# Attention with a two-part fp32r product with V, nine blocks per two heads, six narrow MLP tiles mixed in, written out without loops

## The reference

```python
scores = scale * np.matmul(q, k.transpose(0, 1, 3, 2))
thresh = np.max(scores, axis=-1, keepdims=True) - tau
scores = np.where(scores >= thresh, scores, -1000000000.0)
scores = scores - np.max(scores, axis=-1, keepdims=True)
attn = np.exp(scores)
attn = attn / (np.sum(attn, axis=-1, keepdims=True) + 1e-09)
out = np.matmul(attn, v)
# x: [2304, 512]
h = x @ w_in;  g = h * np.clip(h + 3.0, 0.0, 6.0) / 6.0;  x = g @ w_out
h = x @ w2_in; g = h * (1.0 / (1.0 + np.exp(-1.702 * h))); out = g @ w2_out
```

## Time and profile before

| | before |
|---|---|
| median of 3 runs | 1230.28 us |
| profiled execution, its span | 1225.6 us |
| PE busy (modelled ends) | 1184.3 us, 97% |
| PEld busy | 1020.1 us, 83% |
| DVE busy | 525.8 us, 43% |
| ACT busy | 563.2 us, 46% |
| POOL busy | 545.1 us, 44% |
| chain that ended last | PE 86%, DVE 4%, ACT 4%, issue 4% |
| PE's first product | 11.5 us |
| the first tile behind the attention | from 524.8 us |

### The profile page before, as it was taken

One profiled execution on the slowest core, in us unless ns is written; L12 is line 12 of the kernel. 1 busy time (PEld: TensorE's weight loads), 2 busy tenths in 40 slices (PEclk: granted clock), 3 DMA queues, 4 the chain that ended last, 5 costly groups with the idle time before them and its releaser, 6 DMA issues.

```text
span 1225.6 us, 19677 instructions
## 1 busy us (share of the span) xinstructions
PE 1184.3 (97%) x6408; PEld 1020.1 (83%) x6408; DVE 525.8 (43%) x1344; ACT 563.2 (46%) x1002; POOL 545.1 (44%) x457
## 2 busy tenths in 40 slices
PE   5999999989998999989999999999999999999998
PEld 3666677757776677789999999999999999999997
DVE  5777765576656766332222222222222322222221
ACT  5888765566645765444323333233333222222221
POOL 5888655456645565345333333224444222222222
PEclk9999999999999999999999999999999999999999
DMA  4333322141222312323233322112222112222210
GB/s 121 93 103 111 85 58 60 30 118 49 58 58 68 94 35 58 88 68 120 86 113 111 111 102 81 42 57 72 86 86 86 52 52 78 78 77 77 77 52 26
DMA packets 69736, 94.29 MB, mean 77 GB/s; under 512 B 24368, under 2 KB 45872, under 8 KB 69680
## 3 DMA queue, kind: packets, MB, share of 16 engines
q1 hardware_dynamic: 69680, 93.62, 24.8%
HBM read 70.01 MB, written 23.59 MB: 76 GB/s over the span
## 4 chain that ended last, share of the span: by engine, by line
PE 86%; DVE 4%; ACT 4%; issue 4%; POOL 0%; DMA 0%; DVEq 0%; ACTq 0%; SPq 0%; POOLq 0%
PE mm L417 19%; PE score L429 16%; PE tr L417 14%; PE score L427 12%; PE mm L403 10%; PE score L381 5%; PE tr L389 5%; PE mm L427 5%; ACT expd L663 2%; DVE neg_max L537 2%; DVE prob L551 1%; ACT w_hi L684 1%; ACT gate L702 1%; DVE act_f L580 1%; ACT x_hi L698 0%
## 5 line engine op out<-in xcount | busy, mean ns | idle before, releaser
L814 POOL TENSOR_TENSOR g_lo<-act_f,g_hi 128x384 fp32r<-128x384 f32 x192 | 193.8, 1014 | 442.8 <-ACT g_hi L710 442.8
L803 POOL TENSOR_TENSOR prob<-prob,inv_total 128x576 f32<-128x576 f32 x160 | 183.3, 1148 | 179.5 <-DVE inv_total L565 179.1
L403 PE MATMUL mm<-pt,v_raw 128*64 128x320 f32 (+1 forms) x640 | 182.4, 416 | 4.3 <-ACT o_t L678 4.3
L669 ACT ACTIVATE pt<-tr 128x640 f32<-128x640 f32 x160 | 112.3, 702 | 101.1 <-PE tr L389 100.1
L417 PE MATMUL mm<-x_hi,w_hi 128*128 128x384 f32 x432 | 149.6, 346 | 5.7 <-DVE x_lo L572 3.1
L551 DVE SCALAR_TENSOR_TENSOR prob<-score,thresh,expd 128x576 f32<-128x576 f32 x160 | 130.2, 813 | 50.4 <-ACT expd L663 43.7
L663 ACT ACTIVATE expd<-score,neg_max 128x576 f32<-128x576 f32 x161 | 118.9, 739 | 57.4 <-DVE neg_max L537 56.2
L417 PE MATMUL mm<-x_hi,w_lo 128*128 128x384 f32 x432 | 144.8, 335 | 0.0
L417 PE MATMUL mm<-x_lo,w_hi 128*128 128x384 f32 x432 | 144.7, 335 | 0.0
L537 DVE TENSOR_REDUCE neg_max<-score 128x1 f32<-128x576 f32 x161 | 121.5, 755 | 38.8 <-PE score L381 38.5
L403 PEld LDWEIGHTS mm<-pt,v_raw 128*64 128x64 f32 x640 | 77.1, 136 | 68.1 <-issue 22.0
(11 more groups left out here) (64 smaller groups left out, 2266.8 us busy)
## 6 DMA issues: line engine op xcount, KB each, us to landing
x_raw<-x_t_scratch SPq DMA_DIRECT2D x24, 768.0 KB, 5.8
q_raw<-in_qT SPq DMA_DIRECT2D x68, 144.0 KB, 2.8
k_raw<-in_kT SPq DMA_DIRECT2D x68, 144.0 KB, 2.9
stage<-in_w_in SPq DMA_DIRECT2D x16, 512.0 KB, 6.4
stage<-in_w_out SPq DMA_DIRECT2D x16, 512.0 KB, 6.5
x_t_scratch<-o_t SPq DMA_DIRECT2D x32, 144.0 KB, 2.4
part_t_scratch<-y_out SPq DMA_DIRECT2D x6, 768.0 KB, 4.2
part<-part_t_scratch SPq DMA_DIRECT2D x6, 768.0 KB, 7.8
```

Of the source, the lines that this page charges most:

```text
L403: m = pe.matmul(pv_out[0:HD, 0:n_q], v_raw[:, par, c, :], pt[:, c, cols], start=c == 0, stop=c == QB - 1)
L669: act.activation(pt[:, :, j * P:j * P + P], turned_p.rearrange("p (c n) -> p c n", c=QB), ACT.Copy).then_inc(pt_copied, 1)
L803: pool.tensor_tensor(p, p, inv_total[:, s % RING:s % RING + 1].broadcast_to([P, S]), ALU.mult).then_inc(norm_done, 1)
L814: pool.tensor_tensor(g_lo[:, c, :], act_f[:, c % 2, :], g_hi[:, c, :], ALU.subtract).then_inc(g_lo_done, 1)
```

## The change

A pair of heads now takes nine slots: blocks 0 to 3 of the first head, one block (MID = 4) that holds the last 64 queries of both heads (eight score products, four of them for each head, since q_sp holds zeros beside each tail), and four blocks of the second head. 144 slots in all (G). What each engine does in slot g:

```diff
-            def prob_v(head, par, group, chunks):
...
-                    m = pe.matmul(pv_out[0:HD, 0:n_q], v_raw[:, par, c, :], pt[:, c, cols],
+            def prob_v(n, low):
+                k, side = n % 4, (n % 4) // 2
+                width = GROUP_COLS[k][1]
+                if not low:
+                    pe.wait_ge(pt_hi_done, group_last(n) + 1)
+                    pe.wait_ge(v_lo_done, 2 * (n // 4) + side + 1)
+                    wait(pe, merged, n)
+                else:
+                    wait_low(pe, group_last(n))
+                for c in range(CHUNKS):
+                    p_part = (pt_hi, pt_lo)[low]
+                    m = pe.matmul(pv_out[:, 0:width], v_hl[:, side, c, :], p_part[:, GROUP_BUF[k], c, 0:width],
+                                  start=not low and c == 0, stop=low and c == CHUNKS - 1)
```

v_hl holds V's high part in 64 columns and its low part in the other 64, so one bank receives both parts for 128 rows. The groups are 256, 320, 320 and 256 queries wide. ScalarE copies the lower half out and VectorE adds it to the upper half (`merge`). The tables say in which slot of a pair (counted on past 8) each group's three steps stand:

```diff
+    PV_HI = {4: 0, 7: 1, 9: 2, 11: 3}
+    PV_LO = {5: 0, 8: 1, 10: 2, 12: 3}
+    MERGE = {6: 0, 9: 1, 11: 2, 13: 3}
+    BY_POOL = (5, 8)
```

PE's program:

```diff
+            for g in range(END):
+                if g + 2 < G:
+                    scores(g + 2)
+                if 0 <= g - 2 < G:
+                    turn(g - 2)
+                n = at_slot(PV_HI, g)
+                if n is not None:
+                    prob_v(n, False)
+                n = at_slot(PV_LO, g)
+                if n is not None:
+                    prob_v(n, True)
+                if g in PIECE:
+                    mixed_piece(*PIECE[g])
```

VectorE's program:

```diff
+            for g in range(END):
+                done = PIECE.get(g - 1)
...
+                        gated(ti, mix_out, p).then_inc(mix_drained, 1)
...
+                        drain_y(ti, mix_out, (p - FC) // 2).then_inc(mix_drained, 1)
+                if g + 2 < G:
+                    row_max(g + 2)
+                if g + 1 < G:
+                    mask(g + 1)
+                    if (g + 1) % 2:
+                        invert((g + 1) // 2)
+                if 0 <= g - 2 < G and kind(g - 2) not in BY_POOL:
+                    low_turned(g - 2)
+                n = at_slot(MERGE, g)
+                if n is not None:
+                    merge(n)
```

MLP mixing: step 0 is cut into eight tiles of 288 tokens, and six of them run inside, in pieces of 12 products (a chunk of h, or half a y block):

```diff
+    for b in range(1, B):
+        g0, every = BATCH_SLOTS * b + SLOTS + 1, 8 if b + 1 < B else 4
+        for p in range(2 * PIECES):
+            PIECE[g0 + p + p // every] = (2 * (b - 1) + p // PIECES, p % PIECES)
```

More of the change, by code:

```diff
@@ new lines, in pool_blocks, with wait_low, pt_place @@
+        def pool_blocks(x):
+            return sum(kind(y) in BY_POOL for y in range(x))
+        POOLED = [pool_blocks(x) for x in range(G + 1)]
+        def wait_low(eng, x):
+            wait(eng, lo_by_dve, x + 1 - POOLED[x + 1])
+            wait(eng, lo_by_pool, POOLED[x + 1])
+        def pt_place(tile, x):
+            s = kind(x)
+            if s != MID:
+                group, col = PLACE[s]
+                return tile[:, GROUP_BUF[group], :, col:col + P]
+            base = tile[:, 0, :, 2 * P:2 * P + TAIL]
+            after = tile[:, 1, :, 0:TAIL]
+            return bass.AP(tensor=base.tensor, offset=base.offset,
+                           ap=[list(base.ap[0]), list(base.ap[1]), [after.offset - base.offset, 2], list(base.ap[2])])
@@ L584, in drain_y, with low_turned, merge @@
-            def drain_y(step, bank, m, tile):
+            def low_turned(x):
+                dve.wait_ge(pt_hi_done, x + 1)
+                dve.tensor_tensor(pt_place(pt_lo, x), turned_place(x), pt_place(pt_hi, x), ALU.subtract
+                                  ).then_inc(lo_by_dve, 1)
+            def merge(n):
+                width = GROUP_COLS[n % 4][1]
+                dve.wait_ge(o_low_done, n + 1)
+                wait(dve, o_stored[n % 2], 16 * (n // 2))
+                dve.tensor_tensor(o_t[:, n % 2, 0:width], pv_out[0:HD, 0:width], o_low[:, 0:width], ALU.add
+                                  ).then_inc(merged, 1)
@@ L591, in drain_y @@
                 if partial is None:
-                    return dve.tensor_scalar(y_part(y_out, step, m), bank, scale, None, ALU.mult)
-                return dve.scalar_tensor_tensor(out=y_part(y_out, step, m), in0=bank, scalar=scale,
-                                                in1=y_part(part, step, m), op0=ALU.mult, op1=ALU.add)
-            def pair(i, unit, mlp):
-                for s in range(SLOTS):
-                    g = SLOTS * i + s
-                    mask(g, s)
-                    row_max(g + 1, s + 1)
-                    threshold(g + 1, s + 1)
-                    sum_total(g, s)
-                    if mlp is not None:
-                        mlp(s)
-                    invert(g, s)
@@ L621, in _ @@
-            attention(dve, pair, mix)
-            for k in range(KC):
-                low_x(MIXED, k)
-            def tile_body(step, tile, units):
-                base = first_item(step, tile)
+                    return dve.tensor_scalar(y_part(y_out, ti, m), bank, scale, None, ALU.mult)
+                return dve.scalar_tensor_tensor(out=y_part(y_out, ti, m), in0=bank, scalar=scale,
+                                                in1=y_part(part, ti, m), op0=ALU.mult, op1=ALU.add)
+            row_max(0)
@@ L696, in high_x, with high_half_unit @@
+            def high_half_unit(step, u, n):
+                act.wait_ge((win_loaded, wout_loaded)[n], 16 * (UNITS * step + u + 1))
+                col = n * UNITS * UNIT + u * UNIT
+                act.activation(w_hi[step % 2][:, col:col + UNIT], stage[:, n, :], ACT.Copy).then_inc(w_hi_done, 1)
+            def high_x(ti, k):
+                width = TILES[ti][2]
                 if k == 0:
[L697 to L698 removed]
@@ L700, in gates @@
-            def gates(step, bank, c):
+                    act.wait_ge(x_loaded, 16 * (ti + 1))
+                act.activation(x_hi[:, k, 0:width], x_raw[:, k, 0:width], ACT.Copy).then_inc(x_hi_done, 1)
+            def gates(ti, bank, c):
+                step, _, width = TILES[ti]
                 if step < 2:
-                    act.activation(gate[:, c % 2, :], bank[:, 0:TT], ACT.Relu, bias=three[:, :]
+                    act.activation(gate[:, c % 2, 0:width], bank[:, 0:width], ACT.Relu, bias=three[:, :]
@@ L782, in _ @@
+                high_g(ti, FC - 1)
+                if ti + 1 < len(TILES):
+                    for k in range(KC):
+                        high_x(ti + 1, k)
+                for n in range(2):
+                    if ti == MIXED:
+                        high_half_unit(1, 2, n)
+                    if step > 0 and t < UNITS and step + 1 < STEPS:
+                        high_half_unit(step + 1, t, n)
         @block.gpsimd
@@ L835, in mix @@
-            def mix(tile, s):
-                if s in SPLIT_G:
-                    low_g(SPLIT_G[s], tile)
-            attention(pool, pair, mix)
-            def tile_body(step, tile, units):
-                for c in range(FC):
-                    low_g(c, tile)
-                for unit in units:
-                    for n in range(2):
-                        low_unit(step + 1, unit, (step + 1) * UNITS + unit, n)
-            for step in range(STEPS):
-                tiles_of(pool, step, tile_body)
+            low_q(0)
```

984 lines of the change are left out of this document (513 added, 471 removed).

## The result

| | before | after |
|---|---|---|
| median of 4 runs each | 1230.45 us (1229.63 to 1230.89) | 1394.12 us (1390.92 to 1395.94) |
| ratio | | 1.133, 95% interval 1.131 to 1.135 |
| span of the profiled execution | 1225.6 us | 1389.0 us |
| Pool busy | 545.1 us, 44% | 731.4 us, 53% |

A forecast was written before the change was run, and what follows sets the result against it. TensorE was taken as the bound, except VectorE's chain in attention slots without MLP work. Terms 14.5, 149, 434, 30, 60.6 and 600.7 gave 1289 us of span; with 4.7 for the median, 1293 us, 5% slower, range 1240 to 1335.

The forecast's parts named there:

- bare slots: Slots 0 to 45 of the attention, without MLP work: 13 with the wait at 4.7, 33 at 2.65, 149 us.
- mixed slots: Slots 46 to 143 of the attention, with MLP pieces mixed in: four kinds of slot, together 434 us.
- to the first narrow tile: Slots 144 to 157: 11 MLP pieces, the last turns and PV, three drains of one bank: 30 us.
- two narrow tiles: Two MLP tiles behind the attention: 51.1 us, and 9.5 of stalls while step 1's weights are staged, 60.6 together.
- steps 1 to 3: MLP steps from the fourth tile's start to the end, untouched by the change: 600.7 us.
- The wait: TensorE's high products with V wait for VectorE's merge of the group before, on one bank: 2.7 us in 45 places.
- the clock: Rival: waits drop TensorE to 1.2 GHz in bare slots, PE work doubles: 50 us more, 1343 us; chance 0.08.
- the trace of before speaks against it: Argument against the lower clock: the granted clock is 1.00 in every stage of the kernel before.
- the terms 6.6, 4.7 and 3.7: Length in us of mixed slots: 6.6 with wait and MLP piece, 4.7 with wait alone, 3.7 with piece alone.
- Edits at nothing: Pool's threshold and normalize, unrolling, single q, k, v buffers cost nothing; Pool 28 us a pair against 30, hidden.
- The term of 2.65 us: Slot without MLP work or merge wait, paced by VectorE's sum: about 2.65 us, bounds 2.3 and 3.1.
- The first rival: The merge falls early enough or other slots catch up, so its wait costs nothing: 1179 us, 4% faster; chance 0.15.

The follow-up runs named there:

- fill: Changed kernel plus 20 unread TensorE products of 224 columns ahead of high products that wait for the merge, where the bank is free: 1356.6 us, ratio 1.104.
- merge_first: Changed kernel with VectorE's merge and ScalarE's copy of the lower half at the head of their slots: 1261.0 us, ratio 1.026.
- k_w_moved: merge_first plus one-element sums, broadcast-tensor normalize, step 1 weights staged elsewhere, and k_lo and attention weight splits in other slots: 1221.2 us, ratio 0.992.
- norm_tt: Changed kernel with Pool's normalize as a product with a broadcast tensor instead of tensor_scalar: 1379.3 us, ratio 1.124.
- merge_mid: k_w_moved with VectorE's merge behind the row maximum of block g+2 instead of at the slot's head: 1244.4 us, ratio 1.011.
- merge_norm: merge_first with Pool's normalize as a product with a broadcast tensor: 1263.4 us, ratio 1.028.

## Why the prediction was right in direction and wrong in size

By its own sum, the span (predicted 1289, measured 1389.0):

| stretch | predicted | measured |
|---|---|---|
| to the first mask | 14.5 | 13.7 |
| bare slots | 149 | 188.6 |
| mixed slots | 434 | 490.0 |
| to the first narrow tile | 30 | 32.8 |
| two narrow tiles | 60.6 | 63.2 |
| steps 1 to 3 | 600.7 | 600.7 |

The slots of TensorE by kind tell where the miss lies. Each number is the mean distance, in us, from a slot's first score product to that of the next, read from each trace:

| slots (how many) | predicted | changed kernel | fill | merge_first | k_w_moved |
|---|---|---|---|---|---|
| bare stretch, with the wait (13) | 4.7 | 6.41 | 6.74 | 4.31 | 3.98 |
| bare stretch, others (33) | 2.65 | 3.27 | 3.15 | 3.66 | 3.13 |
| mixed stretch, wait and piece (23) | 6.6 | 7.95 | 6.96 | 3.78 | 3.85 |
| mixed stretch, wait, no piece (9) | 4.7 | 6.18 | 5.82 | 3.99 | 4.20 |
| mixed stretch, piece alone (60 of 62) | 3.7 | 3.90 | 3.71 | 3.88 | 3.70 |

**What held.** The wait: 2.7 us in 45 places forecast, 2.9 in 47 measured. Low part of PT 0.83 against 0.813, merge 0.46 against 0.476 and 0.410. The untouched steps, the drain, and nearly the stalls in the narrow tiles (12.1 us for 9.5), where the chain shows the transfer, twice, and Pool's split behind one g_lo and ahead of the next, as forecast (pieces picked):

```profile
726.52 6.50 DMA stage<-in_w_in
734.90 0.81 POOL g_lo L854
735.71 2.36 POOL w_lo L848
788.25 4.16 PE mm L444 x24
```

**The mixed slots, 56 us over: the clock was left out.** The step that failed is "the trace of before speaks against it", by which the terms 6.6, 4.7 and 3.7 all stood at the full clock. The forecast for these slots, 434 us, comes near fill, in which the wait stands and the clock is nearly full (451.7); the other 38 us of the 490.0 are the clock. The 23 slots with wait and piece show it best. Their high products start 4.39 us behind the slot's first score product in the mean, near the forecast (4.0, and 0.2 in the mean for the MLP drain). From there to the next slot it takes 3.56 us where I had 2.44, and 2.56 in fill. I had given the clock a chance of 0.08 and a price in the bare slots alone; in the mixed slots it cost 38 us. The evidence against it was a clock of 1.00 in a kernel whose TensorE was 94 to 96% busy, and a single idle of 3.13 us. Neither says what repeated waits do. The rule of the Trainium skill (TensorE: Matmul & The Clock Gate, "A second HAM failure mode: psum-queue depth-cycling") that I had weighed and set aside is borne out in kind by these traces: behind such an idle the products lie 0.24 us apart, some microseconds later 0.13, and the mean clock of the stretch is 0.86. The 18 us between the forecast and fill are 10 in the nine slots with the wait and no piece and 8 in those with both.

**The bare slots, 40 us over: other waits were put at nothing.** Both terms failed, 4.7 us for 13 slots with the wait (about 22 us) and 2.65 us for 33 others (about 20 us; the borders of these slots differ a little from those of the masks). Both let TensorE wait for nothing but the merge, and took VectorE's sum as the length of the other slots. In the changed kernel TensorE waits for the merge for 33.8 us up to 203 us; in the same stretch it waits 13.7 us for Pool's k_lo (without the first 10.7), 11.4 for VectorE's low part and 6.8 for the mask. The high products of a slot with the wait start 5.35 us behind its first score product, not 4.0.

Of this excess the runs explain a part. The sum plus 1e-9 had no price of its own; it takes 0.63 us in every second slot, and up to 1.97. With it in one-element operations the high products start at 4.72 us and the bare slots are 10.6 us shorter. "Edits at nothing" was wrong too, in its upper end. Normalize was bounded by its 1.15 us in another form of instruction, and took 1.77; the threshold, taken at 0.2, took 0.294. For nine blocks this is 9 x 0.62 + 9 x 0.09 = 6.4 us more, and 28 us of Pool a pair become 34, against the 30 that I took a pair to last (the terms listed there add up to 22.6 and 27.4, not 22.9 and 28). In the changed kernel this hid behind the longer slots, as norm_tt shows with its 4 us. The condition stood in the text ("if the wait is not there, Pool comes near being the bound"), and it came true: in merge_first the bare slots take 176.7 us, against my 149 with the wait. What the lower clock costs in the changed kernel's bare slots stays open: behind the merge its products take 1.07 us to the next slot, and 0.82 in fill.

The term of 2.65 us for a normal bare slot was too small in every run: the lowest mean is 3.03, in merge_mid. I had named 3.1 us as the point from which I am wrong. Why it can't be had at VectorE's sum is only partly known. No engine sets it alone in k_w_moved, and VectorE is busy for 111.2 of its 155.0 us there. So the step that failed is to price that slot by one engine's sum when it goes round through four.

**The first rival, 1179 us if the wait costs nothing, isn't borne out.** With the wait at 25.7 us and the other faults mended, k_w_moved takes 1221.2. The mixed slots fit the rival's own terms roughly (85 x 3.7 and 13 x 2.65 are 349; 364.1 measured), the bare ones don't (122 for 155.0). In this order the merge waits at the head of VectorE's slot for ScalarE's copy (62.1 us in all); behind the maximum, TensorE waits for the merge instead. What bounds the bare slots in k_w_moved is settled only so far: it isn't Pool's sum, and more clock brought nothing one version earlier. Whether a second bank for the products with V would free both orders was not tried; the eight banks are given out.

**Where the 164 us went.** Step by step from the changed kernel: merge at the head 133, the sum in one-element operations 4, normalize and the weights of step 1 together 16, order of k_lo and the weight splits 19: 173 in sum, which ends 9 us below the kernel before. The shares depend on the order of the steps: alone, the sum is worth 17 us and normalize 15. The 133 are the wait and the clock together; fill puts at least 38 of them on the clock.

## What to carry to other kernels

When a change shares one PSUM bank among successive groups, write out the full order of the engine that frees it and count everything ahead of the freeing step; moving two short instructions to the head of their slots gave 133 us back here. A wait that recurs on TensorE all through a stretch must be priced with the clock as well: here it cost most where TensorE sets the pace. Where four engines wait for each other in a ring, one engine's sum is not the length of a slot: no run came below 3.03 us for the 2.65 forecast. An instruction's price holds for its form alone: before taking over a duration, check that it is the same operation with the same kinds of operands, and that nothing beside it can block it.

## What the runs showed of the hardware

- **Clock.** One idle of 3.13 us ahead of 524.82 us in the kernel before left the products at the pace of 2.4 GHz. In the kernel after, with 47 idles of 2.9 us in the mean over 680 us, the granted clock is 0.81 to 0.86, and products right behind such an idle run at the pace of 1.2 GHz in the rows shown. Products that only fill the idle time raised it to 0.96 in the mixed slots and saved 38 us. In the bare slots it is 0.83 in merge_first too, where these waits are nearly gone: TensorE is busy for 97 of 149 us there.
- **Pool's multiplication with a scalar per row** takes 1767 ns for 576 elements; the product of two tensors, one of them a broadcast of the same column, 1157. The Trainium skill (GPSIMD Engine Reference, 4.1 Engine selection) has one-input operations near line rate and two-input ones about twice as slow as on VectorE, by which the first form would be the cheaper. These runs show the opposite, and the measurement decides.
- **VectorE blocked by Pool.** A VectorE operation on two numbers per partition takes 630 ns in the mean in the kernel after and 2.29 us in merge_norm's row, and its long cases end with Pool's operation beside it. On one number it takes 149 ns, all 144 times together 15.5 us. This agrees with the Trainium skill (SBUF — State Buffer, "Who interferes with whom"): the two engines share a port pair, and while an instruction of one holds it (on VectorE one in a mode that uses both of its port pairs), the other stands still. That it is the ports is the page's explanation; the rows show only that the one ends with the other, and that two elements are enough for it.
